# Strassen products of a two-stage attention and mixture kernel: the first product copied by ACT into the PSUM bank that later products add to, another product order in two steps, and the casts of two units in earlier slots

## The reference

```python
for t in range(S):
    m_new = np.maximum(f_gate[:, :, t] + m, i_gate[:, :, t])
    ...
    C = f_stab[:, :, None, None] * C + i_stab[:, :, None, None] * np.einsum('bhd,bhe->bhde', vt, kt)
    n = f_stab[:, :, None] * n + i_stab[:, :, None] * kt
    ...
    y[:, :, t] = o * h_tilde / denom
...
for e in range(E):                 # E = 4, x is 1536 x 320, w1[e] 320 x 1024, w2[e] 1024 x 320
    h = np.maximum(x @ w1[e], 0.0)
    out += p[:, e:e + 1] * (h @ w2[e])
```

## Time and profile before

| | us |
|---|---|
| median of 3 runs | 413.55 |
| lowest, highest | 411.77, 414.32 |
| the profiled execution | 412.83 |
| its span, first to last instruction | 410.9 |
| mean granted TensorE clock in it | 0.996 of full speed |

### The profile page before, as it was taken

How to read it: one execution, slowest core, us unless ns; L and a number is a source line. 1 busy time by engine, 2 the same in 40 slices (tenths; PEclk the granted TensorE clock), 3 DMA queues, 4 the chain that set the end, 5 groups by cost and what they waited for, 6 DMA issues and landing times.

```text
span 410.9 us, 7284 instructions
## 1 busy us (share of the span) xinstructions
PE 403.0 (98%) x2650; PEld 389.8 (95%) x2650; DVE 261.8 (64%) x490; ACT 192.0 (47%) x378; POOL 193.2 (47%) x227
## 2 busy tenths in 40 slices
PE   8999999999899999999999999999999999999997
PEld 8899999999899999999999999979999999999997
DVE  5885786759444538346249893668665666667654
ACT  4575478659242548434125442344553345434420
POOL 4865835487940558821602001567435643556300
PEclk9999999999899999999999999999999999999999
DMA  7889929684970606341016002222012211230002
GB/s 265 283 283 391 381 92 346 234 284 159 369 274 2 225 2 228 116 176 48 2 30 140 0 2 83 85 84 85 12 73 83 83 29 57 83 101 17 0 2 96
DMA packets 18052, 54.48 MB, mean 133 GB/s; under 512 B 2177, under 2 KB 8850, under 8 KB 16866
## 3 DMA queue, kind: packets, MB, share of 16 engines
q1 hardware_dynamic: 17442, 52.63, 36.8%
q10 hardware_dynamic: 576, 1.40, 1.0%
HBM read 50.40 MB, written 2.05 MB: 128 GB/s over the span
## 4 chain that ended last, share of the span: by engine, by line
PE 94%; DVE 4%; issue 1%; ACT 0%; POOL 0%; DVEq 0%
PE acc_ps L1611 21%; PE hid_ps L1592 21%; PE acc_ps L1677 16%; PE out_ps L1548 5%; PE hid_ps L1677 3%; PE acc_ps L1592 2%; PE out_ps L1655 2%; PE out_ps L1656 2%; PE out_ps L1654 2%; PE out_ps L1653 2%; PE out_ps L1555 2%; PE hid_ps L1441 1%; PE score_ps L1492 1%; PE score_ps L1655 1%; PE add_ps L1655 1%; PE add_ps L1656 1%
## 5 line engine op out<-in xcount | busy, mean ns | idle before, releaser
L1149 DVE SCALAR_TENSOR_TENSOR h_lo<-hid_ps,h_hi 128x384 fp32r<-128x384 f32 (+1 forms) x70 | 35.9, 513 | 84.6 <-ACT h_hi L809 84.3
L809 ACT ACTIVATE h_hi<-hid_ps 128x384 fp32r<-128x384 f32 (+1 forms) x70 | 31.8, 455 | 108.6 <-PE hid_ps L1592 108.5
L1611 PE MATMUL acc_ps<-w_hi,h_hi 128*128 128x320 f32 x208 | 66.4, 319 | 2.5 <-DVE y_acc L1169 2.2
L1611 PE MATMUL acc_ps<-w_hi,h_lo 128*128 128x320 f32 x208 | 64.4, 310 | 0.0
L1611 PE MATMUL acc_ps<-w_lo,h_hi 128*128 128x320 f32 x208 | 64.2, 308 | 0.0
L1592 PE MATMUL hid_ps<-xt_hi,w_hi 128*128 128x384 f32 (+1 forms) x210 | 57.1, 326 | 0.1
L1592 PE MATMUL hid_ps<-xt_hi,w_lo 128*128 128x384 f32 (+1 forms) x210 | 56.6, 324 | 0.0
L612 POOL TENSOR_TENSOR w_lo<-w_raw,w_hi 128x384 fp32r<-128x384 f32 x40 | 45.1, 1131 | 23.5 <-ACT w_hi L795 23.4
L682 POOL TENSOR_TENSOR w_hi<-w_raw,w_hi 128x640 fp32r<-128x640 f32 x12 | 19.6, 1634 | 53.1 <-ACT w_hi L852 53.1
L1611 PEld LDWEIGHTS acc_ps<-w_hi,h_hi 128*128 128x128 f32 x208 | 39.5, 190 | 2.8 <-DVE h_lo L1149 2.7
L676 POOL TENSOR_TENSOR left_lo<-w_raw,left_hi 128x384 fp32r<-128x384 f32 x12 | 13.2, 1101 | 56.6 <-ACT left_hi L835 56.6
(11 more groups left out here) (251 smaller groups left out, 996.6 us busy)
## 6 DMA issues: line engine op xcount, KB each, us to landing
w_raw<-in_w_b SPq DMA_DIRECT2D x19, 704.0 KB, 7.3
w_raw<-in_w_s SPq DMA_DIRECT2D x12, 832.0 KB, 4.6
raw<-in_qk_s SPq DMA_DIRECT2D x8, 1024.0 KB
g_all<-g_dram SPq DMA_DIRECT2D x10, 512.0 KB, 6.9
kv<-in_kv_n SPq DMA_DIRECT2D x12, 352.0 KB, 6.1
q_pack<-in_q_p SPq DMA_DIRECT2D x10, 192.0 KB, 6.9
out_y<-y_acc SPq DMA_DIRECT2D x12, 160.0 KB, 1.8
carry<-g_dram SPq DMA_DIRECT2D x30, 60.0 KB
```

Source lines behind the costliest of these rows:

```text
L809: nc.scalar.activation(h_hi[:, M % RING, 0:cols], hid_bank(M)[:, 0:cols], ACT.Relu).then_inc(hid_hi, 1)
L1149: nc.vector.scalar_tensor_tensor(h_lo[:, M % RING, 0:cols], hid_bank(M)[:, 0:cols], 0.0, h_hi[:, M % RING, 0:cols].bitcast(fp32), ALU.max, ...
L1611: last = nc.tensor.matmul(acc_ps[t][:, 0:DM], x, w, start=(f == 0 and i == 0), stop=(f == NF - 1 and i == 2))
```

## The change

- **Casts.** For units 6 and 7 the slots of `CAST` and `SUB` are earlier: unit 6 casts in 19, 20 and subtracts in 20, 21; unit 7 casts in 25, 26 and subtracts in 27, 29.
- **Product 1.** `keep_1`, `add_2`, `add_3` and `add_21` go. ACT's `spread_1` copies product 1 from `score_ps` into `out_ps`, and product 6 no longer opens the bank: it adds to the copy, and 7 and 4 add further. ACT takes over the copies to `sum_2` and `sum_3` (`keep_2`, `keep_3`). Product 6 now waits for the copy. One matmul of 128x512 into `out_ps` is added ahead of product 1 of step 0; every later product 6 finds the bank as the step before left it.
- **Order.** Step 1 has the product order (1, 6, 7, 4, 2, 5, 3), with its four down products after the first three and the sixth; step 11 has (1, 6, 5, 7, 4, 2, 3). In both, block 21 is taken before block 11.
- ACT's and DVE's programs around steps 1 and 2 are rewritten to suit.

```diff
-CAST = {4: (11, 12), 5: (16, 17), 6: (24, 25), 7: (28, 30), 8: (35, 37), 9: (41, 43), 10: (44, 47), 11: (51, 52)}
-SUB = {4: (13, 14), 5: (18, 19), 6: (26, 27), 7: (30, 32), 8: (37, 38), 9: (43, 45), 10: (46, 48), 11: (53, 54)}
+CAST = {4: (11, 12), 5: (16, 17), 6: (19, 20), 7: (25, 26), 8: (35, 37), 9: (41, 43), 10: (44, 47), 11: (51, 52)}
+SUB = {4: (13, 14), 5: (18, 19), 6: (20, 21), 7: (27, 29), 8: (37, 38), 9: (43, 45), 10: (46, 48), 11: (53, 54)}
...
+SECOND_ORDER, LAST_ORDER = (1, 6, 7, 4, 2, 5, 3), (1, 6, 5, 7, 4, 2, 3)
+SECOND_DOWNS = (0, 1, 2, 5)
...
+            def spread_1(t):
 
                 act.wait_ge(product_done, product_count(t, 1))
...
+                wait_if(act, low_of[21], t)
+                nc.scalar.activation(out_ps[:, 0:width(t)], score_ps[:, 0:width(t)], ACT.Copy).then_inc(kept_1_done, 1)
+
+            def keep_2(t):
+
+                act.wait_ge(product_done, product_count(t, 6))
+                wait_if(act, whole_of[12], t)
+                nc.scalar.activation(sum_2[:, 0:width(t)], out_ps[:, 0:width(t)], ACT.Copy).then_inc(sum_2_done, 1)
+
+            def keep_3(t):
+
+                act.wait_ge(product_done, product_count(t, 7))
+                wait_if(act, whole_of[22], t)
+                nc.scalar.activation(sum_3[:, 0:width(t)], out_ps[:, 0:width(t)], ACT.Copy).then_inc(sum_3_done, 1)
...
-            keep_1(1)
+            spread_1(1)
             wide_relu(0, 12)
-            for t in range(1, STEPS):
-                if t > 1:
-                    keep_1(t)
+            keep_2(1)
+            own_highs(2)
+            keep_3(1)
+            sums_highs(2)
+            wide_relu(0, 22)
+            wide_relu(1, 21)
+            wide_relu(1, 11)
+            step_down_high(2)
+            keep_5(1)
+            wide_relu(1, 12)
+            wide_relu(1, 22)
+            for t in range(2, STEPS):
+                spread_1(t)
                 if t + 1 < STEPS:
                     own_highs(t + 1)
                     sums_highs(t + 1)
+                keep_2(t)
                 keep_5(t)
...
+                keep_3(t)
+                for c in blocks_of(t):
+                    wide_relu(t, c)
...
                     if t == 0:
                         pe.wait_ge(rest_low, 1)
                         pe.wait_ge(p_ready, 2 * NT)
+                        pe.wait_ge(xt_done, NT)
+                        nc.tensor.matmul(out_ps[:, :], left_lo[:, 0, 0, :], xt_hi[:, 0, 0:WIDE], start=True, stop=True)
...
-                    wait_if(pe, low_of[21], t)
+                    pe.wait_ge(kept_1_done, t + 1)
...
-                nc.tensor.matmul(to, hi[:, 0:128], x_hi, start=m in (1, 5, 6), stop=False, skip_group_check=True)
+                nc.tensor.matmul(to, hi[:, 0:128], x_hi, start=m in (1, 5), stop=False, skip_group_check=True)
```

More of the change, by code:

```diff
@@ L286, in build @@
                 "g": fresh[0:U0, L:2 * L] if n == 0 else row(17, r), "j": row(at, r),
-                "gg": (sb("gg0", [U0, 2 * L])[:, :] if n == 0 else row(at + 3, r, 2)).rearrange("u (t l) -> u t l", t=2),
+                "gg": (gg0[:, :] if n == 0 else row(at + 3, r, 2)).rearrange("u (t l) -> u t l", t=2),
                 "w": row(at + 1, r), "key": row(at + 2, r),
@@ L340, in build @@
         sum_2_done, sum_3_done, half_done = sem("sum_2_done"), sem("sum_3_done"), [sem(f"half_done{i}") for i in range(2)]
-        whole_of = {c: sem(f"whole_{c}") for c in (12, 21, 22)}
+        whole_of = {c: sem(f"whole_{c}") for c in (12, 22)}
         high_of, low_of = ({c: sem(f"{x}_{c}") for c in (11, 12, 21, 22)} for x in ("high", "low"))
@@ L1404, in _ @@
             wide_low(0, 12)
-            for t in range(1, STEPS):
+            sums_lows(2)
+            wide_low(0, 22)
+            wide_low(1, 21)
+            step_rest_low(2)
+            wide_low(1, 11)
+            add_12(1)
+            wide_low(1, 12)
+            wide_low(1, 22)
+            for t in range(2, STEPS):
                 add_wide(t, 0)
-                add_2(t)
                 if t + 1 < STEPS:
                     sums_lows(t + 1)
+                    step_rest_low(t + 1)
                 add_wide(t, 1)
-                if t + 1 < STEPS:
-                    step_rest_low(t + 1)
-                if t == 1:
-                    wide_low(0, 22)
-                add_3(t)
                 add_wide(t, 2)
                 add_wide(t, 3)
-                wide_low(t, 11)
-                add_21(t)
-                wide_low(t, 21)
-                add_12(t)
-                wide_low(t, 12)
-                wide_low(t, 22)
+                for c in blocks_of(t):
+                    if c == 12:
+                        add_12(t)
+                    wide_low(t, c)
             for t in range(STEPS, STEPS + 2):
@@ L1735, in _ @@
                 turns = [(half_of, i) for half_of in (ahead, behind) if half_of is not None for i in range(pairs(half_of[1]))]
+                at = SECOND_DOWNS if t == 1 else range(len(turns))
                 for n in range(8):
                     if t < STEPS and n < len(ORDER):
-                        product(t, ORDER[n])
-                    if n < len(turns):
-                        wide_down(*turns[n][0], turns[n][1])
+                        product(t, order_of(t)[n])
+                    if n in at:
+                        half_of, i = turns[at.index(n)]
+                        wide_down(*half_of, i)
 def kernel(**inputs):
```

48 lines of the change are left out of this document (13 added, 35 removed).

## The result

| | before | after |
|---|---|---|
| median of 15 runs each, us | 412.76 | 416.14 |
| lowest, highest | 411.29, 414.32 | 413.93, 418.49 |
| profiled execution, us | 412.83 | 416.62 |
| its span | 410.9 | 414.3 |
| its mean granted clock | 0.996 | 0.991 |

The ratio of after to before is 1.0078, with a 95% interval of 1.006 to 1.0096: the change costs 3.2 us (2.5 to 4.0). The forecast was 412.7 in a range from 410.7 to 415.4, so it missed upwards. It stood on a median of three runs, 413.55; fifteen give 412.76, so the sum of -0.8 us missed by 4 us and not by 3.4.

The account below looks back on a forecast made before the run. PE, busy 98%, was taken as the bound, with about 5 us within reach. Terms -2.1 + 1.5 - 1.7 + 0.2 + 0.6 + 0.5 + 0.4 - 0.2 = -0.8 us gave 412.7 us, range 410.7 to 415.4.

Parts of the forecast that it names:

- the casts: Earlier cast and subtraction slots for units 6 and 7, clock included: -2.1 + 1.5 - 1.7 = -2.3 us.
- the products: Copied product 1 and the new orders of steps 1 and 11: +0.2 + 0.6 + 0.5 + 0.4 - 0.2 = +1.5 us.
- The clock (-1.7): The 3.41 us at half clock from 106.07 us would go, with no new fall: -1.7 us, bounds -1.7 and 0.
- the clock falls after slot 24: Rival: the new 1.5 us wait at slot 24 makes the clock fall there instead; 414.4 us, chance 0.25.
- Slot 24 (+1.5): Before slot 24's down: unit 6's early subtractions delay DVE's evictions 1.76 us; new PE wait +1.5 us, bounds 1.2 and 2.0.
- Slot 32 (-2.1): Before slot 32's down the 2.17 us wait shrinks to 0.4, and slot 30's 0.3 goes: -2.1 us, bounds -2.5 and -1.3.
- The added matmul (+0.2): One more matmul of 512 columns on PE, 0.23 us: +0.2 us.
- Product 6 in the middle steps (+0.6): Steps 1 and 3 to 7: product 6's weight load starts some 0.1 us later, awaiting the copy; +0.6 us, bounds 0 and 1.5.
- the rival of the slow copy: ACT's copy into PSUM is slow and holds up product 6; at 0.3 us longer, +2.7 us, 415.4 us; chance 0.1.
- The 0 that I drew from it: If ACT's way to PSUM is faster, as the skill says, product 6's +0.6 us would be 0.
- Steps 1 and 2 (+0.4): The 0.64 us wait at step 2's first down product goes; product 6 of step 2 waits 1.0: +0.4 us, bounds 0 and +0.8.
- Step 11 (+0.5 - 0.2): Product 6 waits for a late copy, +0.5 us (0.4 to 0.7); the new order removes a 0.24 us wait, -0.2.

Follow-up runs that it names:

- casts_alone: The kernel before with only the change's new cast and subtraction slots for units 6 and 7: 413.59 us against 412.57, ratio 1.0022.
- unit6_early: The kernel before with unit 6 casting in slots 19, 20 and subtracting in 20, 21, unit 7 subtracting in 32, 33: 413.55 us against 412.88, ratio 1.0006.
- unit7_late: The kernel before with unit 7's subtractions in slots 32 and 33 instead of 30 and 32: 410.30 us against 412.57, ratio 0.9948.
- after_u7: The changed kernel with unit 6's old cast and subtraction slots, unit 7 casting in 28, 30 and subtracting in 32, 33: 413.89 us against 412.88, ratio 1.0015.
- turned: unit7_late with product order (1, 6, 5, 7, 4, 2, 3) in steps 1 and 11, product 1 still added by DVE: 410.97 us against 413.32, ratio 0.9951.
- p6_waits: The kernel before with product 6 also waiting for ACT's copy of product 1, still to SBUF: 416.34 us against 412.57, ratio 1.0087.
- step11_plain: The changed kernel with step 11 in the common product order: 416.59 us against 412.57 for the kernel before, ratio 1.0097.
- products_alone: The changed kernel with the old cast and subtraction slots: 416.40 us against 412.57 for the kernel before, ratio 1.0090.
- p5_second: The changed kernel with product 5 ahead of product 6 in steps 2 to 10: 415.93 us against 412.57 for the kernel before, ratio 1.0095.

## Why the prediction was wrong

The sum was -0.8 us; the change costs 3.2. Both halves missed upwards: the casts -2.3 forecast and +0.9 (0.0 to 1.8) measured, the products +1.5 forecast and some 2.9.

**The clock (-1.7): the step that failed most.** It said that a wait of 1.5 us lies between 2.17, with a fall, and 0.64, without, and took no fall. The runs show that the fall is a matter of the execution as well, and not of the kernel alone. Of the 78 executions of the kernel before that ran beside these experiments, 27 had a mean clock of 1.00 (median 411.9 us), 43 had 0.996, which is one fall (413.2 us), and 8 less (415.4). The mean doesn't say where the fall was. So a fall like that of the earlier trace rows is worth 1.4 us and comes in two executions of three, and a term read off one profile had both its size and its certainty wrong. (In the trace it is 1.5 us: while the clock is low, PE's lag behind the kernel before grows from 3.10 to 4.58 us.) Of the kernels with some two microseconds of waiting at slot 24, 10 of 15 executions of the changed one have a mean under 0.999, 8 of 12 of casts_alone, 6 of 12 of unit6_early. With 0.6 us at slot 32 and nothing at slot 24 (unit7_late, after_u7, turned): 2 of 31. The change had to end the long waits to gain the clock and only moved them: it falls in 10 of 15 executions where it fell in 51 of 78, and the gain of 1.7 us is none. Nor is the clock the loss: without a fall the changed kernel takes 415.0 us (5 executions) against 411.9. The rival "the clock falls after slot 24" had the mechanism and the place, with 0.25; by these counts it was the likelier case.

**Slot 24 (+1.5): under-sized, and one consumer missed.** DVE came 2.67 us late and not 1.76. Of the 0.9 us more, 0.4 is ACT's by the rows (no run took it apart): the cast of 1.06 us stands in front of the ReLU that restarts DVE. I had called it free because ACT stood idle for 3.86 us and the DMA engines had gone quiet. But the row of the cast says that it waited for `raw` until 74.27, at the very end of that idle time, and the ReLU's data arrived while it ran. Another 0.5 is stretch, 0.42 us on a `w_lo` that took 0.48 before and 0.90 now (the rows at 77.55 and 81.15), and 0.14 on the next, each beside a POOL instruction of 1 to 2 us. And PE met the delay first at the scores of unit 5, which wait for `prob` from the same DVE queue (0.92 us), then at `down` (1.19). The sum is 2.54 us on PE.

The Trainium skill ("SBUF — State Buffer", section "SBUF: two separate sides") has DVE instructions with two SBUF inputs and POOL's lock each other out, which I priced at up to 1 us and left out of the sum. The trace agrees in kind: beside POOL `w_lo` was stretched, and while the second subtraction was not, at 1.32 us, the POOL instruction that started 0.22 us behind it took 1.98 us where the earlier trace rows have 1.01. That the price gives 2.5 us, just what PE lost, is in part luck: 0.5 us of the miss is stretch, and 0.4 is ACT's cast.

**Slot 32 (-2.1): right.** 2.17 became 0.72, where 0.4 was forecast as left, and the 0.3 of slot 30 went; by PE's starts the two gave 1.97 us.

**The added matmul (+0.2): right**, 0.23.

**Product 6 in the middle steps (+0.6): right**, 0.60 over steps 3 to 7 and 0.12 in step 1; in steps 8 to 10 it was 0.04 where nothing was forecast. p6_waits has the same with an SBUF copy, so this was the wait for the copy, as argued. ACT's copy itself, by group (mean in ns before the idle time):

```profile
L873 ACT ACTIVATE out_ps<-score_ps 128x512 f32<-128x512 f32 x8 | 4.7, 583 | 6.7 <-PE score_ps L1668 6.7
L891 ACT ACTIVATE kept<-add_ps 128x512 f32<-128x512 f32 x8 | 4.8, 596 | 4.9 <-PE add_ps L1668 4.9
```

So the rival of the slow copy falls: 583 ns into PSUM, 596 into SBUF. The Trainium skill ("ScalarE: Activation LUTs", section "Step-by-step: what each stage is for") calls PSUM the faster way; the trace agrees by 13 ns, which is a tenth of the overhang and saved nothing. The 0 that I drew from it did not come.

**Steps 1 and 2 (+0.4): 0.98 with product 6 of step 1, against some 0.5 for both.** The wait of 1.0 us at product 6 of step 2 is as worked out. It costs 1.23 us, and the 0.64 us that goes gives back 0.88 (by the starts in the trace of turned), so the exchange costs the 0.35 us of the sum. Left out were 0.09 us at product 7 of step 2 and, with 0.42 us, the new hand-overs inside step 1: products 7, 4 and 3 now each wait one down product behind a copy, and their first matmul covers 0.30, 0.30 and about 0.34. POOL's `step_down_low` took 1.90 us and not 1.57, within the 0.4 that the prediction allowed for.

**Step 11 (+0.5 - 0.2): 0.64 against 0.3.** The wait was 0.48 as forecast, and 0.72 us with its restart, which the sum did not have. Of the order's 0.24 us only 0.08 came, since 0.15 us behind an eviction stands in its place, as the bound said, and it was no gain of the order: step11_plain has it too.

**Outside the span.** 0.4 us had no term at all. In the kernel before and in all those that keep its products, the time is 1.92 us longer than the span (median of each, 1.91 to 1.93); with the copied product it is 2.2 to 2.4. What does that wasn't tried.

Behind the slots then, 1.5 forecast, 2.5 in the trace, 0.4 outside it: 2.9. By the ratios of three pairs of kernels (products_alone to before, after_u7 to unit7_late, the changed kernel to casts_alone) it is 3.7, 2.8 and 2.3.

## What to carry to other kernels

Moving an accumulation off a side engine buys nothing while PE is the bound, and it costs as soon as PE has to wait for the copy: look at what lies between the copy's source and its first reader (here one down product of 0.88 us, and the copy needs about 1.0 with its hand-overs), and count some 0.2 us more than the idle time for every wait that comes, and as much for one that goes. Work moved out of one full stretch of a side engine belongs behind the deadline that it was holding up, not in front of the one before: here unit 7's subtractions in slots 32 and 33 gained 0.5%, and unit 6's in slots 20 and 21 cost 2.4 us. And before a fall of the clock is booked as gain or loss, take the mean clock of many executions, not the one profile.

## What the runs showed of the hardware that was not expected

- The fall to 0.50 after a wait is not determined by the kernel alone: the same program has it in one execution and not in the next (27 of 78 without). From slot 24 on it came, in the profiles, behind waits of 1.2 to 2.2 us, and p5_second, with 1.1 and 1.2 us at slot 24, had none. Of the 31 executions of the three kernels whose profiles have no wait above 1.0 us from slot 24 on, 2 had a fall; one is the profiled one of turned, and there the clock was low from 39.2 to 42.7 us, right behind the second of two waits of 0.57 us for POOL's `w_lo`. In step11_plain two low stretches followed each other behind slot 24 (clock 0.50 from 86 to 92 us, mean 0.992).
- The first matmul of a product covers 0.24 us more behind a wait: 0.47 for 0.23 at 512 columns, 0.41 for 0.17 at 384. Before a down product a wait of 0.64 us cost 0.88. So the idle time of the timeline is less than what the wait costs.
- The 0.4 us outside the span, above.
